# Where the first early piece of a step stands in the queues of a fused attention and expert kernel

## The reference

```python
scores = scale * np.matmul(q, k.transpose(0, 1, 3, 2))
kth = np.partition(scores, -top_k, axis=-1)[..., -top_k:-top_k + 1]
scores = np.where(scores >= kth, scores, -1000000000.0)
attn = softmax(scores)
x = matmul(attn, v)                      # heads side by side: 512 columns
logits = np.einsum('bsd,de->bse', x, w_gate)
e = argmax(logits[b, s])  or the previous token's e
out[b, s] = p[e] * (np.maximum(x[b, s] @ w1[e], 0.0) @ w2[e])
```

## Time and profile before

| what | value |
|---|---|
| median of 3 runs | 1034.29 us (1033.83 to 1036.27) |
| the profiled execution | 1033.68 us, its span 1031.7 us |
| granted TensorE clock, mean | 0.838 |
| PE, DVE busy | 77%, 74% of the span |
| ACT, POOL busy | 40%, 59% of the span |
| the chain that ended last | PE 21%, from 787 us on |
| eviction of an early piece on ACT (L760 to L784) | 0.60 us each |
| transfer of half of an expert's weights by ACT | 10.7 us to landing, median |
| first expert tile after the attention, L645 | at 793.06 us |

### The profile page before, as it was taken

How to read it: one execution, slowest core, us unless ns; L and a number is a source line. 1 busy time by engine, 2 the same in 40 slices (tenths; PEclk the granted TensorE clock), 3 DMA queues, 4 the chain that set the end, 5 groups by cost and what they waited for, 6 DMA issues and landing times. The chain is left out here.

```text
span 1031.7 us, 15965 instructions
## 1 busy us (share of the span) xinstructions
PE 799.3 (77%) x3928; PEld 454.6 (44%) x3929; DVE 762.4 (74%) x1617; ACT 417.0 (40%) x913; POOL 612.9 (59%) x557
## 2 busy tenths in 40 slices
PE   2566757666766665579989989989746999999996
PEld 1343434443433343345555555545434444444442
DVE  5999999999999998999999999899833111111010
ACT  2445554555545455235555665655520111111110
POOL 0877888788878887478888888798501011111111
PEclk7677686767668687568999999999955999999998
DMA  3091101010010103010541545354400045453610
GB/s 119 1 372 35 49 1 49 14 35 17 31 47 0 47 13 127 14 55 9 223 168 75 221 184 187 111 194 174 174 24 30 21 168 231 175 201 135 240 32 27
DMA packets 17498, 103.96 MB, mean 101 GB/s; under 512 B 2638, under 2 KB 5198, under 8 KB 13328
## 3 DMA queue, kind: packets, MB, share of 16 engines
q1 hardware_dynamic: 10560, 57.68, 15.0%
q10 hardware_dynamic: 3024, 34.19, 8.5%
q0 software_dynamic: 3840, 11.28, 3.1%
HBM read 93.70 MB, written 10.75 MB: 101 GB/s over the span
## 5 line engine op out<-in xcount | busy, mean ns | idle before, releaser
L1194 POOL TENSOR_SCALAR p_sb<-s_sb,top 128x576 f32<-128x576 f32 x141 | 313.7, 2225 | 98.3 <-DVE top L917 95.3
L917 DVE MAX8 top<-work 128x8 f32<-128x576 f32 x432 | 307.0, 808 | 0.0
L395 PE MATMUL ps<-id_sb,p_sb 128*128 128x128 f32 x720 | 130.2, 322 | 180.3 <-ACT p_sb L723 180.3
L925 DVE MATCH_REPLACE8 work<-top,work 128x576 f32<-128x576 f32 x288 | 216.8, 806 | 0.0
L1197 POOL TENSOR_TENSOR p_sb<-p_sb,s_sb 128x576 f32<-128x576 f32 x141 | 198.8, 1410 | 25.9 <-POOL p_sb L1194 23.5
L395 PEld LDWEIGHTS ps<-id_sb,p_sb 128*128 128x128 f32 x720 | 96.3, 165 | 227.9 <-issue 227.9
L1098 DVE TENSOR_SCALAR moe<-ps 128x512 f32<-128x512 f32 x30 | 20.8, 692 | 193.4 <-PE ps L645 193.4
L385 PE MATMUL ps<-qk_sb 64*128 64x288 f32 (+1 forms) x640 | 139.1, 575 | 6.8 <-DMA qk_sb<-in_qk 5.9
L731 ACT ACTIVATE pT_sb<-ps 128x640 f32<-128x640 f32 x144 | 101.3, 703 | 104.1 <-PE ps L395 102.9
L723 ACT ACTIVATE p_sb<-p_sb,nmax 128x576 f32<-128x576 f32 x144 | 110.8, 770 | 76.9 <-POOL p_sb L1197 76.6
L424 PE MATMUL ps<-pT_sb,v_sb 128*64 128x64 f32 (+5 forms) x1152 | 126.2, 383 | 10.3 <-ACT pT_sb L731 10.0
(11 more groups left out here) (140 smaller groups left out, 728.6 us busy)
## 6 DMA issues: line engine op xcount, KB each, us to landing
w_sb<-in_w SPq DMA_DIRECT2D x16, 2048.0 KB, 10.0
w_sb<-in_w ACTq DMA_DIRECT2D x16, 2048.0 KB, 10.7
qk_sb<-in_qk SPq DMA_DIRECT2D x16, 864.0 KB, 4.6
v_sb<-in_v SPq DMA_DIRECT2D x16, 320.0 KB, 2.9
x_dram<-x_sb SPq DMA_DIRECT2D x2, 1024.0 KB, 5.9
x_dram<-x_sb SPq DMA_DIRECT2D x2, 768.0 KB, 4.6
x_dram<-x_sb SPq DMA_DIRECT2D x2, 256.0 KB, 2.4
wg_sb<-in_wg ACTq DMA_DIRECT2D x1, 292.0 KB, 8.0
```

The source lines that it names most:

```text
L395: mm = pe.transpose(ps[:, 2 + c // 4, (c % 4) * P:(c % 4 + 1) * P], p_at(n % GROUP)[:, c * P:(c + 1) * P], id_sb[:, :])
L917: dve.max(top[:, par, j, rnd, :], src).then_inc(chain, 1)
L925: dve.match_replace(work[:, j, :], top[:, par, j, rnd, :], src, NEG).then_inc(chain, 1)
L1194: pool.tensor_scalar(p_at(j)[:, 0:S], s_at(n % RING), top[:, k % 2, j, ROUNDS - 1, 7:8], -BIG, ALU.is_lt, ALU.mult).then_inc(masked, 1)
```

## The change

The slot 0 of a step moves on both engines. On PE it stands behind turn 0, the second scores ahead and the turning back, ahead of turn 1; on ACT behind take_pT 0, exponent 1 and the take of ahead 1, ahead of take_pT 1. All that is in slot 0 moves along: 16 early pieces (q = 5 to 8, 10 to 17, 19 to 22), the placing matmuls of k = 3 in pair 4, and the exponent of the gates of k = 2 in pair 4. DVE, POOL and SP are unchanged.

```diff
@@ tensor engine, step @@
                     ahead(k, 0)
                     if k > 0 or not first:
                         values(*before(r, k))
-                    slot(r, k, 0)
                     turn(r, GROUP * k)
                     ahead(k, 1)
                     if k > 0 or not first:
                         turn_back(*before(r, k))
+                    slot(r, k, 0)
                     turn(r, GROUP * k + 1)
                     ahead(k, 2)
                     slot(r, k, 1)
```

## The result

The changed kernel took 1060.19 us (median of 4 runs, 1058.53 to 1063.50), the kernel before 1034.06 beside it: a ratio of 1.0253 with a 95% interval of 1.0222 to 1.0284. The forecast was 1059.7. The profiled execution was the slowest of the four, 1063.50 us with a span of 1061.5, so it holds 29.8 us more than the profiled one before, where the medians differ by 26.1.

What follows compares the result with a forecast made beforehand. DVE's 48 steps bound the kernel, nearly co-bound by PE's queue. 5.5 + 4.4 + 14.8 + 0.7 = 25.4 us on 1033.68 gives 1059.1, and 1059.7 us as median (2.5% slower), range 1043 to 1071.

Steps and rivals of the forecast that it cites:

- What bounds the kernel: DVE's 48 steps of 14.5 us set the time, co-bound with PE's queue of about 15 through the third score eviction.
- Part 1: Pair 4, k = 2: DVE waits longer at L959 for the gates' exponent moved later on ACT, +5.5 us.
- Part 2: Pair 4, k = 3: DVE waits for the placing matmuls, now behind PE's turning back and taking 1.28 us, +4.4 us.
- Part 3: Early pieces: 1.50 us PE hole ahead of turn 0 in 15 steps, less covered waits and slack, +14.8 us.
- rival B: The holes make PE's clock fall, 3 us per lapse: 1075 us with five lapses, 1105 with 15; chance 0.15.
- The drain: The slot 0 piece of q = 22 delays turn 2 of that step and all that follows, +0.7 us.
- The sum: 5.5 + 4.4 + 14.8 + 0.7 = 25.4 us more, 1059.1 for the profiled execution, 1059.7 for the median.
- A: PE's holes ahead of turn 0 stay hidden and only the routing waits and the drain show: 1044.9 us; chance 0.14.
- C: ACT reaches exponent 1 and the second eviction earlier, DVE's 6.4 us of waits go: 1028 us at best; chance 0.03.
- D: Nothing measurable: the routing waits are made up later and the holes hidden; chance 0.03.

Runs made afterwards that it cites:

- experiment 9: The changed kernel with an extra 507-column ACT copy between values' eviction and exponent 0, in the 16 steps with a slot 0 piece: 1096.19 us, ratio 1.0607.
- 10: The kernel before with the same extra 507-column ACT copy, pieces in their old place: 1033.32 us, ratio 1.0005.
- Experiment 3: The kernel before with only the gates' exponent on ACT moved behind exponent 1 and the second take: 1039.57 us, ratio 1.0067.
- experiment 12: The kernel before with early pieces moved, exponent 0 ahead of the values' eviction on ACT, and the gates' exponent ahead of exponent 0: 1020.32 us, ratio 0.9881.
- Experiment 5: The changed kernel with exponent 0 ahead of the eviction of the values on ACT: 1035.97 us, ratio 1.0054.
- experiment 1: The kernel before with only the early pieces moved, routing work in its old place on both engines: 1048.07 us, ratio 1.0149.
- 8: The kernel before with only ACT's evictions of the slot 0 pieces moved behind exponent 1 and the second take: 1032.99 us, ratio 0.9990.
- 11: The changed kernel with a shorter extra ACT copy (128 columns) between values' eviction and exponent 0, in steps with a slot 0 piece: 1063.51 us, ratio 1.0286.

## Why the prediction was right, by its own steps

**What bounds the kernel.** Right. Experiments 9 and 10 show it from both sides: time added on ACT where PE waits for it ahead of turn 0 goes into the total one for one and more, the same time where PE has the piece to do does not.

**Part 1, the gates' exponent.** Right in mechanism and size: the wait came out at 9.23 us, 5.4 more than before, and the step grew by 5.1 (forecast 5.5). DVE's own work behind the wait changed in both directions: L962 took 1.36 us instead of 0.23, the scan at L979 and L980 together 1.1 less. That this nearly cancels is luck. Experiment 3 has it alone; experiment 12, which moves it the other way, removes the wait.

**Part 2, the placing matmuls.** Right in mechanism; the term was too small, 6.0 measured for 4.4. I took the duration from where the matmuls stood before, behind the values and at the upper level of the clock. In the new place, behind 8 us of idle and in a step whose turn takes 1.30 us, they run at the lower level (clock 0.50): 2.21 for 1.28. The row to take the level from was that of the neighbours in the new place; the 1.55 us of the turning back in the earlier trace rows showed it. The other 0.7 us is L995.

**Part 3, the holes.** Right. I wrote 1.50 us for each; the trace has 1.48 to 1.50. The waits ahead of turn 1 fell away as listed, and PE's idle time in the stretch grew by 15.2 us, where the chain with its slack gave 14.8. Experiment 5 took the cause away and the holes with it. What the sum lacked is 2.5 us of slow clock, a small piece of rival B. The four runs of the changed kernel spread over 5 us (0.5%) where those before lie within 3. The one with the lowest mean clock (0.819) is the slowest, but the other three do not go by their clocks (0.823, 0.831 and 0.828 for 1059.06, 1058.53 and 1061.32 us), so that the clock makes the spread is a guess.

**The drain.** 1.5 for 0.7, and not by the forecast path. Turn 2 of q = 22 does wait 2.04 us behind the piece, but it starts 10.75 us after the values of its step (769.42 - 758.67) where that was 10.48 before: 0.3 us, not 0.7. The other 1.2 us are the clock. Turn 0 of q = 23, which waits 1.49 us in both, ran at the upper level before and at the lower one after, and the values of the last two steps took 3.47 and 3.63 us instead of 3.29 and 3.18. First before, then after:

```profile
746.50 0.74 PE L395 MATMUL ps<-id_sb,p_sb 128*128 128x128 f32 x5 [1.49 <-ACT p_sb L723]
753.10 3.18 PE L424 MATMUL ps<-pT_sb,v_sb 128*64 128x256 f32 x36
```
```profile
766.68 0.71 PE L395 MATMUL ps<-id_sb,p_sb 128*128 128x128 f32 x5
769.42 0.74 PE L395 MATMUL ps<-id_sb,p_sb 128*128 128x128 f32 x5 [2.04 <-ACT p_sb L723]
...
776.01 1.30 PE L395 MATMUL ps<-id_sb,p_sb 128*128 128x128 f32 x5 [1.49 <-ACT p_sb L723]
...
783.17 3.63 PE L424 MATMUL ps<-pT_sb,v_sb 128*64 128x256 f32 x36
```

**The sum** was 25.4 for a difference of medians of 26.1. Part of that closeness is luck: 29.8 us separate the two profiled executions, and the terms for placing, clock and drain were too small by 1.6, 2.5 and 0.8, with 0.4 more idle time; 0.3 us were lost before any of it; 0.4 too much in part 1 and 0.8 us won in the expert tiles (a wait of 1.02 us for weights before is absent after) go the other way.

**The rivals.** A (holes hidden) is out by experiment 1. C (faster) is out by 8. D (nothing measurable) is out by the result. B had 0.15 and came about only in traces of it; experiment 9 shows how near it was. Two things in B were not as the rows have them. PE's queue did have holes before, one of 3.88 us at q = 18, and the piece behind that one took 4.77 us. And a lapse of the clock cost less than the 3 us put there: 25.2 us of busy time for ten more slow steps than before in experiment 9, 2.5 us for two more in the changed kernel.

## What to carry to other kernels

Before moving filler work in an in-order queue, ask of both places which wait it covers there: the old place hid a chain of two instructions on another engine (1.5 us), the new one mostly only 0.2 us, and the difference was paid in each step that the queue bounded. Look too for the rare passengers of the same slot; two one-off pieces of work (one exponent and twelve small matmul records) cost 11 of the 29.8 us here. And when a hole opens, look whether the chain behind it can be put in another order (here two instructions on ACT) before giving up the move.

## What the runs showed of the hardware

- The clock of TensorE does not answer to a hole in proportion. PE's busy time for the 1340 records of the stretch was 238.19 us before the change; with holes of 1.49 us in 15 steps it was 240.71 and 241.92 (the changed kernel and experiment 1), with 1.69 us 242.05, with 2.00 us 263.39. In two of these, experiments 1 and 11, one hole of the 15 was longer, 2.08 and 2.19 us. Single holes do not decide it by their length alone: in the kernel before, the clock fell behind 1.82 us at q = 9 and not behind 1.48 at q = 18, and in experiment 9 it held behind 1.82 us at q = 9 and behind three of the 2.00 us. The Trainium skill ("TensorE: Matmul & The Clock Gate", section "A second HAM failure mode: psum-queue depth-cycling") names short idles between groups of matmuls as a cause of such swings. These runs agree for 2.00 us and show that 1.49 mostly does not do it here.
- A DVE instruction with two operands in SBUF (L995, 128 x 72) took 0.93 us instead of 0.23 beside another POOL instruction than before. Here POOL had L1197 (two tensors) under way, and L995 ended 0.09 us after it; in the kernel before POOL had L1194 (one tensor). L962, also with two operands, shows the same: it starts while L1197 runs and ends 0.09 us after it. The rows of the changed kernel:

```profile
418.53 1.36 DVE L962 TENSOR_TENSOR gates<-lexp,linv 128x72 f32<-128x72 f32 x1
...
418.40 1.40 POOL L1197 TENSOR_TENSOR p_sb<-p_sb,s_sb 128x576 f32<-128x576 f32 x1 [0.18 <-POOL p_sb L1194]
...
450.13 1.40 POOL L1197 TENSOR_TENSOR p_sb<-p_sb,s_sb 128x576 f32<-128x576 f32 x1 [0.18 <-POOL p_sb L1194]
```

The Trainium skill ("GPSIMD Engine Reference", section "1. Specifications") says that GpSimd's SBUF access is shared with VectorE, with contention where a DVE instruction has two SBUF inputs. The slow cases fit that. That the same two instructions took 0.23 us beside L1194 is not explained by it. Which of POOL's instructions matters was not tried.
